# First batch's inverse with T and M in one product and Q by whole transposes; reciprocal and key scaling half a period ahead; three buffers for EA

## What is computed

```python
for t in range(S):
    y[:, :, t] = np.einsum('bhd,bhde->bhe', rt, state)
    Sa = np.einsum('bhde,bhe->bhd', state, at)
    state_decay = state * wt[:, :, None, :] - np.einsum('bhd,bhe->bhde', Sa, bt)
    state = state_decay + np.einsum('bhd,bhe->bhde', vt, kt)
...
x = _moe_ref(x=x, **moe_kwargs)
return _moe2_ref(x=x, **moe2_kwargs)
```

## Time and profile before

| | |
|---|---|
| runs | 1173.79, 1174.92, 1187.32 us; median 1174.92 |
| the profiled execution | 1171.18 us, span 1169.4 us |
| PE / DVE / ACT / GpSimd busy | 1032.0 / 539.3 / 398.5 / 325.1 us |
| instructions | 53,687 |
| lone stage of the recurrence | 0 to 214.3 us |
| recurrence beside mixing and attention | 214.3 to about 960 us |
| last attention alone | about 960 us to the end |

### The profile page before, as it was taken

The page is one execution under the profiler, slowest core; times in us unless marked ns, Lnnn a source line. Parts: engine busy times, 40 slices in busy tenths (PEclk is TensorE's granted clock), DMA queues, the critical chain, the costliest instruction groups (busy, mean ns, idle before and its releaser), DMA issues. The chain is left out here.

```text
span 1169.4 us, 53687 instructions
## 1 busy us (share of the span) xinstructions
PE 1032.0 (88%) x24432; PEld 764.6 (65%) x24432; DVE 539.3 (46%) x1152; ACT 398.5 (34%) x1069; POOL 325.1 (28%) x588
## 2 busy tenths in 40 slices
PE   4777767899999897899999898799999897899978
PEld 4766666666776776666766676666666686655556
DVE  5554445334335775233434767414334675210274
ACT  2333333322223454423223455432212454310155
POOL 4544444332223432122322433212322420000000
PEclk9998999999999999899999999899999999999989
DMA  6232232233122221112111212101111111000000
GB/s 203 69 93 83 84 100 83 73 99 105 45 61 59 72 75 47 53 39 61 48 57 46 82 52 77 61 28 46 51 54 39 48 54 33 27 1 1 1 12 24
DMA packets 48001, 68.52 MB, mean 59 GB/s; under 512 B 19744, under 2 KB 34848, under 8 KB 47776
## 3 DMA queue, kind: packets, MB, share of 16 engines
q1 hardware_dynamic: 47776, 65.09, 18.5%
HBM read 57.19 MB, written 7.86 MB: 56 GB/s over the span
## 5 line engine op out<-in xcount | busy, mean ns | idle before, releaser
L488 POOL TENSOR_TENSOR QI<-R,consts 128x256 f32<-128x256 f32 x240 | 173.9, 735 | 458.9 <-DVE R L656 420.9
L656 DVE COPY R<-PB 128x512 f32<-128x512 f32 x147 | 100.9, 686 | 172.7 <-PE PB L914 170.6
L550 ACT COPY R<-PB 128x512 f32<-128x512 f32 x147 | 86.5, 588 | 217.7 <-PE PB L914 215.8
L906 PEld LDWEIGHTS PB<-R 64*64 64x64 f32 x5376 | 96.6, 138 | 70.2 <-issue 54.8
L906 PE MATMUL PB<-R 64*64 64x64 f32 x5376 | 117.0, 227 | 23.2 <-issue 7.5
L1135 PE MATMUL PB<-uf,W 128*128 128x384 f32 x320 | 111.5, 494 | 0.6 <-issue 0.6
L1167 PE MATMUL PB<-work,W 128*128 128x384 f32 x320 | 107.2, 488 | 1.4 <-issue 0.7
L1135 PEld LDWEIGHTS PB<-uf,W 128*128 128x128 f32 x320 | 58.1, 190 | 46.1 <-issue 12.1
L914 PE MATMUL PB<-R,QI 64*64 64x64 f32 x3072 | 77.3, 221 | 12.1 <-issue 11.8
L1167 PEld LDWEIGHTS PB<-work,W 128*128 128x128 f32 x320 | 59.4, 190 | 40.1 <-DVE work L831 1.3
L831 DVE TENSOR_SCALAR work<-PB 128x384 f32<-128x384 f32 x40 | 22.3, 558 | 124.6 <-PE PB L1142 73.4
(11 more groups left out here) (136 smaller groups left out, 1885.6 us busy)
## 6 DMA issues: line engine op xcount, KB each, us to landing
EA<-ea_dram SPq DMA_DIRECT2D x48, 498.0 KB, 3.6
LA<-la_dram SPq DMA_DIRECT2D x48, 384.0 KB, 3.4
VT<-vt_dram SPq DMA_DIRECT2D x48, 80.0 KB, 1.8
x_mid_dram<-XO SPq DMA_DIRECT2D x192, 20.0 KB, 1.9
xs<-x_mid_dram SPq DMA_DIRECT2D x24, 160.0 KB, 3.2
out_dram<-work SPq DMA_DIRECT2D x24, 160.0 KB, 2.1
W<-w_dram SPq DMA_DIRECT2D x7, 320.0 KB, 4.4
W<-w_dram SPq DMA_DIRECT2D x1, 1280.0 KB, 8.5
```

Of the source, the lines that this page charges most:

```text
L488: nc.gpsimd.tensor_tensor(QI[j][:].rearrange("p (u g t) -> p u g t", u=2, g=2), src.rearrange("p u (g t) -> p u g t", g=2), eye3.unsqueeze ...
L550: freed(nc.scalar.copy(tile[:, 8 * C:16 * C], PB[PLACE[group, i][0]][:, 1, :]), group, i)
L656: freed(nc.vector.tensor_copy(tile[:, 0:8 * C], PB[PLACE[group, i][0]][:, 0, :]), group, i)
L906: mm = nc.tensor.matmul(out[half(m1), u, col:col + C], left, right, start=True, stop=True)
```

## The change

**The first batch's inverse.** For chunks 0 to 11 (`turned`) the other algorithm runs. M and T stand beside each other in one tile (`with_sums`), and `double` multiplies both by T at once: eight products with 128 columns instead of 16 squares and 8 extensions with 64. The left side Q is no longer computed but turned: `turn_back` transposes the whole T part with two 128x128 transposes per round (steps `t1` to `t4`), DVE and ACT copy the blocks out into `QI`, four half-height copies per step. GpSimd adds the old M to the new product (`add_up`, `first_sum`), where it made `QI` and `M1` before. The last rounds are `last_parts`. ACT's copies of bank 1 swap halves and so are two of 64 partitions each.

```diff
+            def double(out, Q, R, lo):
+                for g, p, u in HEADS:
+                    new = out[half(p ^ u), u, 2 * C:6 * C].rearrange("p (x g t) -> p x g t", x=2, g=2)[:, :, g]
+                    mm = nc.tensor.matmul(new, Q[half(p), (2 * u + g) * C:(2 * u + g + 1) * C],
+                                          with_sums(R, lo)[half(p), u, :, g], start=True, stop=True)
+                return mm
+
+            def turn_back(out, bank_, R, lo):
+                per = R.shape[1] // 2
+                for u in range(2):
+                    mm = nc.tensor.transpose(out[:, bank_, u * P:(u + 1) * P], R[:, u * per + lo:u * per + lo + P], ident)
+                return mm
...
             def round2(n, out):
+                if turned(n):
+                    taken(pe, "t1", n)
+                    pe.wait_ge(sum_made[1], n + 1)
+                    return double(out, QI[1], R1, 0)
                 taken(pe, "r1", n)
                 return square(2, out, 0, R1, 0)
...
+            def add_up(j, what, n, here, before):
+                taken(pool, what, n)
+                nc.gpsimd.tensor_tensor(here, here, before, ALU.add).then_inc(sum_made[j], 1)
+                pool.wait_ge(sum_made[j], n + 1)
...
+                if any(flips):
+                    lo, hi = columns(group, i) if all(flips) else (6 * C, 8 * C)
+                    for p in range(2):
+                        freed(nc.scalar.copy(tile[half(p), 8 * C + lo:8 * C + hi], ps[half(1 - p), 1, lo:hi]), group, i)
...
+                elif what in ("T42", "T31"):
+                    is_full(dve, what, n)
+                    for x in members_of(what, n):
+                        for p in range(2):
+                            freed(nc.vector.tensor_copy(of_heads(QI[int(x[1])], p, 0),
+                                                        in_block(turned_in(x, PB[PLACE[what, n][0]]), p, 0)), what, n)
```

```diff
-BK_DEPTH, PT_DEPTH, END_DEPTH, AF_DEPTH, VT_DEPTH, VK_DEPTH, OB_DEPTH = 5, 5, 5, 4, 4, 3, 3
+BK_DEPTH, PT_DEPTH, END_DEPTH, AF_DEPTH, VT_DEPTH, VK_DEPTH, OB_DEPTH = 5, 6, 5, 5, 4, 3, 3
+EA_DEPTH = 3
-LEAD = {"scan": 2, "bk": 1, "den": 2, "inv": 2,
+LEAD = {"scan": 3, "bk": 2, "den": 2, "inv": 2,
-PERIOD = ("bk", "A1", "A2", "A3", "scan", "mix", "B1", "B2", "B3", "mix", "den", "C1", "C2", "inv", "C3", "mix")
+PERIOD = ("A1", "A2", "A3", "mix", "B1", "B2", "B3", "mix", "den", "C1", "C2", "inv", "scan", "C3", "mix", "bk")
+LAST_PERIOD = ("A2", "A1", "A3", "T42", "B3", "den", "B2", "inv", "B1", "C4", "C1", "C2", "C3", "scan", "bk")
+FIRST_PERIOD = ("A3", "B3", "scan", "B4", "den", "A1", "B1", "C2", "T42", "B2", "inv", "bk", "A2", "C1", "C4", "C3", "T31")
-        EA, LA, VT = ring("EA", 2, EA_COLS), ring("LA", 2, LA_COLS), ring("VT", VT_DEPTH, TOK)
+        EA, LA, VT = ring("EA", EA_DEPTH, EA_COLS), ring("LA", 2, LA_COLS), ring("VT", VT_DEPTH, TOK)
...
             load_vt(0)
+            load_ea(2)
```

More of the change, by code:

```diff
@@ L73, in drains_of @@
         i, = args
[L74 to L77, removed]
+        ops = {"U": 1, "o2": 1, "X": 1, "o3": 1, "s2": 1, "s1": 3, "s3": 2, "ST": 1, "o1": 2,
+               "t1": 4, "t2": 4, "t3": 4, "t4": 4}
+        if what in ("A1", "B1", "C1"):
+            flips = flips_of(what, i)
+            return 2 if not any(flips) else 3 if all(flips) else 4
+        if what == "A2":
+            return 4 if turned(chunk_of("r1", i)) else 2
+        return sum(ops[x] for x in members_of(what, i))
     if what in ("score", "h", "qk", "v"):
@@ L319, in program @@
         qi_made = {j: sem(f"qi_made{j}") for j in range(1, 6)}
+        sum_made = {j: sem(f"sum_made{j}") for j in range(1, 7)}
         stored = [sem(f"stored{j}") for j in range(2)]
@@ L444, in _ @@
                     sp.dma_start(WO[:], t["wo"].rearrange("(j p) n -> p j n", p=P)).then_inc(rest_in, 16)
-                elif what == "C2" and chunk_of("ST", i) is not None:
+                elif what in ("C2", "C4") and "ST" in members_of(what, i):
                     n = chunk_of("ST", i)
@@ L449, in _ @@
                         load_vt(n + VT_DEPTH)
-                elif what == "B2" and chunk_of("o3", i) is not None:
+                elif what in ("B2", "B4") and "o3" in members_of(what, i):
                     n = chunk_of("o3", i)
@@ L570, in _ @@
                     second("C1", n, R36)
+                elif what in ("T42", "T31"):
+                    is_full(act, what, n)
+                    for x in members_of(what, n):
+                        turned_back((what, n), int(x[1]), turned_in(x, PB[PLACE[what, n][0]]))
+                elif what == "A2" and turned(chunk_of("r1", n)):
+                    is_full(act, "A2", n)
+                    src = PB[PLACE["A2", n][0]][:, 1, 0:2 * C].rearrange("p (g t) -> p g t", g=2)
+                    for p in range(2):
+                        freed(nc.scalar.copy(with_sums(R1, 0)[half(p), 1, 0], src[half(1 - p)]), "A2", n)
                 elif what == "A2":
@@ L575, in _ @@
                     freed(nc.scalar.copy(at(VK, n)[:], ps[:, 0, 4 * C:4 * C + TOK]), "A2", n)
-                elif what == "B2" and chunk_of("X", n) is not None:
+                elif what == "B2" and "X" in members_of("B2", n):
                     is_full(act, "B2", n)
@@ L655, in first @@
                 is_full(dve, group, i)
-                freed(nc.vector.tensor_copy(tile[:, 0:8 * C], PB[PLACE[group, i][0]][:, 0, :]), group, i)
+                lo, hi = columns(group, i) if all(flips_of(group, i)) else (0, 8 * C)
+                freed(nc.vector.tensor_copy(tile[:, lo:hi], PB[PLACE[group, i][0]][:, 0, lo:hi]), group, i)
             def scan(n):
```

259 lines of the change are left out of this document (186 added, 73 removed), and 2 rows, old and new, of the table LEAD.

## The result

The changed kernel takes 1168.82 us (median of 20 runs, 1159.50 to 1175.63), the kernel before beside it 1175.68 us (20 runs). The ratio is 0.9941, interval [0.9918, 0.9964]: 7 us faster, where the forecast said 25 us, and within the 2% that this measurement tells from no change. 1168.8 lies above the top of the range, 1165. The profiled execution took 1174.32 us.

What follows compares the result with a forecast made beforehand. PE's instruction packets were taken to bound the lone stage: 1171.2 - 3.5 (first periods) - 28.3 (fewer packets) + 6.5 (new chain's waits) = 1145.9 us. The runs' median lies 3.7 us higher, so 1150 us, range 1139 to 1165.

Steps and rivals of the forecast that it cites:

- Packets bound the lone stage: Ahead of the mixing, PE's instruction fetch sets the time: about 256 instructions a packet, 3.93 us each; 9.7 packets go.
- Columns: In the inverse's 128-column products, rows take 30 ns; a period's column work stays 7.8 us, so columns give nothing.
- First periods: Start of the lone stage, bound by the chain, not packets: ends at 38.0 us, gain 3.5 us, between 0 and 9.8.
- The rest of the lone stage: After the first periods, up to the mixing: 7.2 packets fewer save 28.3 us, less 6.5 us given back.
- the give-back: Lone stage's full periods: waits of the new chain not hidden cost 0.65 us each, 6.5 us over ten periods.
- the walk: A full lone-stage period traced without stops: 9.75 us, DVE some 8.2 us busy, PE waiting 2.0 us; packets want 10.6.
- my own sign: Stated test for the lone stage: packets further apart than 4.3 us would mean the forecast is wrong and the chain rules.
- The chain takes over: Rival, lone stage: dearer copies or late sums make periods 12.6 us, 20 us given back, 1163 us; chance 0.20.
- Beside the mixing: In 33 periods after the lone stage, the scan's move costs 0, between -2.8 and +36 us; instruction count stays.
- DVE's block beside the mixing: Rival: reciprocal, scan and product delay A1's copy in each of 33 periods, up to 36 us, 1186 us; chance 0.06.
- The sum: Whole kernel: 1171.2 - 3.5 - 28.3 + 6.5 = 1145.9 us as profiled, 1149.6 or 1150 us as median of runs.

Runs made afterwards that it cites:

- e4: The changed kernel once more, nothing altered, for a second profile: 1167.25 us, ratio 0.9909 to the kernel before.
- e1: The changed kernel with the scan beside mixing and attention moved back ahead of B1's group, still 3 chunks ahead: 1153.27 us, ratio 0.978 to the kernel before.
- e8: The changed kernel with the scan beside the mixing behind C3's group instead of ahead of it: 1155.77 us, ratio 0.9828 to the kernel before.
- e5: The kernel before with the scan and its product right behind the reciprocal from period 15 on, one Af buffer more: 1191.34 us, ratio 1.0136.
- e9: The changed kernel with the scan beside mixing and attention behind B2's group: 1152.05 us, ratio 0.9829 to the kernel before.
- e10: e9 with the reciprocal beside the mixing moved behind C3's group too: 1152.09 us, ratio 0.9824 to the kernel before.
- e11: A repeat of e1 for a second profile: 1151.86 us, ratio 0.9831 to the kernel before.
- e6: The kernel before with 24 unread products of 2 columns added per lone-stage period, 96 instructions a period: 1194.41 us, ratio 1.0147.

## Why the prediction was wrong

**Packets bound the lone stage: right.** Counted 9.7 packets fewer, ten came in all, nine of them ahead of the mixing. The instruction experiment gives 4.04 us a packet: 24 small products a period, without columns to speak of, cost 21.2 us. The Trainium skill, in "Runtime: NRT & Kernel Launch", section "Instruction fetch mechanics", calls the crossing from block to block mostly hidden; the 21.2 us, and the stops of the earlier trace rows, say that here it is not.

**Columns: right.** Forecast 30 ns for a row of 128, measured 30.7.

**First periods: right.** The transposes of `s1` that stood at 41.5 us stand at 38.1; 38.0 had been worked out.

**The rest of the lone stage: the give-back was mis-sized.** "I take 0.65 us a period, bounds 0 (all hidden) and 2.0 (none)" put 6.5 us against 28.3. From 38.1 us to the end the stage took 162.8 us for the 151 forecast and the 173.8 of before: 11.0 us gained, so 17.3 of the 28.3 were given back, 1.7 us for each of the ten periods. The full periods alone account for 1.5: in four profiles they take 12.1 us in the mean, where I had 11.25 and packets alone want 10.6. Where the remainder goes, these rows don't tell. The two periods at full clock above, 11.5 and 11.3 us, are what I forecast, and PE's waits ahead of T42 and T31 (line 1063) stay at 0.5 us or under. DVE's busy time there, 9.0 to 9.2 us, is more than the 8.2 of the walk, and what that costs no run shows. The rest goes with the clock. Of 32 full periods in four profiles with this lone stage (the changed kernel, e4, e1 and e8; from one pair of `s1`'s transposes to the next), 21 with at most 2 us at 1.2 GHz are 11.4 us long in the mean, the other 11 13.4 us, and a straight line through all gives 0.41 us more for each microsecond at 1.2 GHz. Before, periods with and without it were about equally long (14.0 and 13.8 us, 16 periods in the profiles of before and e5). My reading, argued from these lengths and tested by no run alone: the slower columns ran inside the stops for instructions; with 208 of 897 instructions gone, much of that cover is gone too. I had counted "the stretches at a clock of 1.2 GHz" into the 0.65 without pricing them. By my own sign, packets further apart than 4.3 us, the chain now rules, with the clock: 37 packets in 162.8 us are one each 4.4. The amount given back lies nearer to the 20 us of the rival "The chain takes over" than to my 6.5, but the undisturbed periods of 11.4 us are not its 12.6. Over the seven profiles with this lone stage (these four, e9, e10 and e11) it ends between 195.7 and 206.2 us, mean 200.5, so the stage gives about 15 us.

**Beside the mixing: this step failed.** "After the reciprocal DVE was idle for 1.64 us before its next work, which covers the 1.1 us. I take 0" rests on one place, at 257 us, in the mixing. A hundred microseconds on, in the attention, the work behind the reciprocal is the softmax's scaling, and PE waits for it. Instead of 0 the move costs 14 to 15 us (e1 against e4, e5 against its kernel before). The rival "DVE's block beside the mixing" had the mechanism and held the price within its bound of 36 us, but it named the wrong victim (A1's copy) and asked for a wait in each of 33 periods. Neither is so: from the mixing's first product to 1010.6 us (988.8 in e1), PE's wait for line 955 is the first row below in the changed kernel, and the second in e1.

```profile
PE PB L1425 <- DVE work L955: 7.2, 4, 2.5
```

```profile
PE PB L1425 <- DVE work L955: 2.9, 3, 2.5
```

That is 4.3 us more. The waits for `SS` on line 1074 grew from 1.3 to 3.5 us and those for a round's copy on lines 1157 and 1170 from 3.6 to 5.2 us: some 8 us in all. The kernel pays 14 us, and the profiles differ by 37.8 us at 1.2 GHz, so the other 6 us are put down to the clock, by the argument above. Chunk by chunk the changed kernel falls behind e1 around these places: the five periods from the wait on are 8.9 us longer in the first attention (112.2 for 103.3) and 7.8 in the second (108.6 for 100.8), and the seven periods between them are equal within 0.1 us. I had read no wait through the clock at all.

**The sum.** 1175.7 - 15 (lone stage) = 1160.7, and 14 to 15 for the scan make some 1175; measured were 1168.8. The 6 us between are open: with the scan undone the kernel is 21 to 24 us faster than before, some 6 to 9 us more than the lone stage shows. The one profile of the kernel before had a granted clock of 0.975, where its runs have 0.963 in the mean, so that profile shows less of the time at 1.2 GHz than a typical run spends. The profiles don't tell where in the program those runs lose it.

The Trainium skill, in "TensorE: Matmul & The Clock Gate", section "Part 1: The HAM clock gate (the "warmup" mystery)", ties the clock to how busy PE has been. The traces agree where PE stops more: 0.81 in the lone stage of e6 for 0.96 before, and stretches at 1.2 GHz at all twelve long waits; the 7 of 27 places without such a wait show that this wait is not all that the clock follows. The same section of the Trainium skill puts the penalty of the warm-up ramp under 1% of a typical span; here the move of one scan cost 1.2% (14.0 of 1167 us), by waits and clock together.

## What to carry to other kernels

Where tiles are small, count PE's instructions: in the lone stage of the kernel before 256 of them took 4 us, and still did with wide or with tiny products added. Price a DVE instruction that moves in every stage that it runs beside, and first in the one where another's short chain passes through the same queue; an idle time behind it in one stage covers nothing in the next. And count a new wait of PE, even one of 1.5 us, at more than its length: the period that held it here was 5.2 us longer.

## What was not expected of the hardware

All twelve waits of 1.36 to 1.64 us at the attentions' first scaled weights stood beside a stretch at 1.2 GHz of 3.4 to 10.2 us; with a wait of at most 0.20 us at the same place 7 of 27 did. While instruction packets set the pace, periods with time at 1.2 GHz were no longer than others (14.0 and 13.8 us); in the new lone stage they were longer by 0.41 us per microsecond. The rows of products of 2 columns started 29 ns apart (e6), hardly closer than the 30.7 ns of the rows of 128 columns on line 1056. Work added to PE for nothing went with a higher mean clock over the runs: 10 us more in the lone stage, 3 us over the whole kernel (1180.61 against 1177.54).
